# Attention in steps of four heads instead of two, with the PSUM banks, the rings of q and k and the place of the transposes rearranged, in an attention + MLP + experts kernel

## The reference

```python
# 1. attention with a causal window of 128 and a linear bias for each head
scores = q @ k.T / sqrt(64)
rel = pos[:, None] - pos[None, :]
scores = where((rel >= 0) & (rel < 128), scores - slope[h] * abs(rel), -1e9)
attn = exp(scores - max(scores)); attn /= sum(attn) + 1e-9
x = attn @ v                                   # 2304 x 512
# 2. MLP, d_ff = 2048
h = x @ w_in
x = (h * clip(h + 3, 0, 6) / 6) @ w_out
# 3. each token goes to one of 8 experts (cosine similarity with an embedding), d_ff = 1024
out[t] = gate[t] * (max(x[t] @ w1[e], 0) @ w2[e])
```

## Time and profile before

| | |
|---|---|
| three runs | 952.06, 955.26, 955.92 us |
| the profiled execution | 952.92 us, of which the span from first to last instruction is 951.2 us |
| PE busy | 898.1 us (94%) |
| DVE busy | 505.7 us (53%) |
| ACT busy | 439.2 us (46%) |
| POOL busy | 233.4 us (25%) |
| granted TensorE clock, mean | 0.991 of full |
| first `up` of the MLP | 35.67 us from the start of the span |
| last `values` of the attention | 552.44 us |

### The profile page before, as it was taken

How to read it: one execution, slowest core, us unless ns; L and a number is a source line. 1 busy time by engine, 2 the same in 40 slices (tenths; PEclk the granted TensorE clock), 3 DMA queues, 4 the chain that set the end, 5 groups by cost and what they waited for, 6 DMA issues and landing times.

```text
span 951.2 us, 17668 instructions
## 1 busy us (share of the span) xinstructions
PE 898.1 (94%) x5821; PEld 745.7 (78%) x5821; DVE 505.7 (53%) x1537; ACT 439.2 (46%) x1203; POOL 233.4 (25%) x247
## 2 busy tenths in 40 slices
PE   5799999899999999999999999799999999999996
PEld 3678888787788887787888889676788888888885
DVE  6755448566566665565665554678355345435100
ACT  4577545454445544545545433372344333344441
POOL 5464000000000000000000010036556556655532
PEclk9899999999999999999999999999999999999999
DMA  8542411101211101112100000366545544543100
GB/s 188 135 133 74 144 34 34 45 7 24 57 34 34 45 8 45 34 35 56 23 7 23 1 24 1 113 198 203 173 128 166 178 123 146 185 128 112 38 22 10
DMA packets 83415, 75.39 MB, mean 79 GB/s; under 512 B 61736, under 2 KB 61736, under 8 KB 83202
## 3 DMA queue, kind: packets, MB, share of 16 engines
q1 hardware_dynamic: 78754, 61.94, 22.9%
q0 software_dynamic: 4000, 11.29, 3.8%
q10 hardware_dynamic: 576, 1.05, 0.4%
HBM read 64.80 MB, written 11.30 MB: 80 GB/s over the span
## 4 chain that ended last, share of the span: by engine, by line
PE 87%; DVE 5%; ACT 2%; issue 2%; DMA 1%; POOL 1%; POOLq 0%; SPq 0%; ACTq 0%; DVEq 0%
PE ps_h L712 21%; PE ps_y L727 20%; PE ps_h L831 14%; PE ps_s L864 14%; PE ps_s L663 4%; PE ps_stage_out L696 4%; PE ps_t L675 4%; PE ps_y L855 2%; PE ps_stage_out L647 1%; PE ps_t L804 1%; ACT gated_hi L985 1%; DVE dot_junk L1170 1%; DVE arena L1130 1%; DMA arena<-in_k 1%; DVE row_den L1139 1%
## 5 line engine op out<-in xcount | busy, mean ns | idle before, releaser
L712 PE MATMUL ps_h<-x_hi,win_hi 128*128 128x256 f32 x576 | 175.3, 304 | 1.6 <-DVE x_lo L1159 1.6
L712 PE MATMUL ps_h<-x_lo,win_hi 128*128 128x256 f32 x576 | 164.0, 285 | 0.0
L712 PE MATMUL ps_h<-x_hi,win_lo 128*128 128x256 f32 x576 | 163.9, 285 | 0.0
L1191 DVE TENSOR_TENSOR gated_lo<-gated,gated_hi 128x256 fp32r<-128x256 f32 x144 | 62.9, 437 | 132.5 <-ACT gated_hi L985 132.1
L985 ACT CAST gated_hi<-gated 128x256 fp32r<-128x256 f32 x144 | 58.4, 406 | 153.9 <-PE ps_y L727 135.2
L981 ACT ACTIVATE clip<-ps_h,half 128x256 f32<-128x256 f32 x144 | 68.6, 476 | 121.4 <-PE ps_h L712 121.0
L727 PE MATMUL ps_y<-wout_hi,gated_hi 128*128 128x512 f32 x288 | 115.0, 399 | 2.1 <-issue 2.1
L712 PEld LDWEIGHTS ps_h<-x_hi,win_hi 128*128 128x128 f32 x576 | 111.0, 193 | 5.1 <-DVE x_lo L1159 2.0
L543 POOL MEMSET arena<- 128x128 bf16 x1 | 0.2, 204 | 464.9 <-DVE x_lo L1159 464.9
L727 PE MATMUL ps_y<-wout_hi,gated_lo 128*128 128x512 f32 x288 | 113.9, 396 | 0.0
L727 PE MATMUL ps_y<-wout_lo,gated_hi 128*128 128x512 f32 x288 | 112.5, 391 | 0.0
(11 more groups left out here) (197 smaller groups left out, 1729.4 us busy)
## 6 DMA issues: line engine op xcount, KB each, us to landing
arena<-in_moe_w SPq DMA_DIRECT2D x64, 512.0 KB
y_scratch<-y_sb SPq DMA_DIRECT2D x9, 512.0 KB, 3.7
arena<-in_v SPq DMA_DIRECT2D x16, 256.0 KB, 2.9
en_all<-in_moe_w_out SPq DMA_DIRECT2D x16, 256.0 KB, 2.8
arena<-in_q SPq DMA_DIRECT2D x15, 256.0 KB, 3.2
arena<-in_k SPq DMA_DIRECT2D x15, 256.0 KB, 3.9
en_all<-in_moe_w_in SPq DMA_DIRECT2D x12, 256.0 KB, 3.1
en_all<-en_scratch SPq DMA_DIRECT2D x1, 2048.0 KB, 10.0
```

What stands on the lines that cost most here:

```text
L712: last = pe.matmul(ps_h[m % 2][:, 0:TB], a[:, c, w], r[:, c, x], start=n == 0, stop=n == 3 * KC - 1)
L1191: dve.tensor_tensor(gl[m % 2][:], gate[:], gh[m % 2][:], ALU.subtract).then_inc(dve_gl, 1)
```

## The change

A step is now one group and four heads (`q4`, half of the eight): 40 steps instead of 80.

- **Banks.** The staged heads fill the bank `ps_stage` (four transposes), the outputs have the bank `ps_out` (256 columns). The transposes of `prob`, now two banks full, go into the banks of the scores, `ps_s` (in the first four steps into the MLP's `ps_h`). So `values` no longer waits for the stage copy, nor `stage` for `x_lo`; `scores(s)` waits for `take_pT(s-2)` and `transposes(s)` for DVE to have read the scores of step s + 1.
- **Depth.** `OUT` is 2 instead of 3 and `prob` has two buffers instead of three. `transposes(it-1)` stands in the same iteration as `normalise(it-1)`; before, it was one iteration behind it.
- **Order.** From iteration 5 (the new `FIRST`) to 40 there are 3.5 slots to an iteration: 16 of 3, 16 of 4, and one each of 1, 2, 5 and 6. PE does `values`, `scores`, two slots, `transposes`, `stage`, the other slots. DVE does one slot (with its router passes) ahead of `normalise`. ACT does two exponentials, a slot, two exponentials, a slot, and then `take_pT` and `stage_copy`. In iterations 0 to 4 PE does `values(it-2)`, `scores(it)`, `stage(it+1)`, `transposes(it-1)`.
- **Loads.** q and k come four heads at a time into rings of three. POOL splits two weight pieces for each normalised step instead of one. The embedding's small work moves to iterations 7 and 10.

```diff
-    STEPS = NG * NP
+    NQ = NP // 2
+    STEPS = NG * NQ
-    NEGS, OUT = 3, 3
+    OUT = 2
...
-    EMB_AT, EN_AT = FIRST + 4, FIRST + 8
-    EARLY = FIRST - OUT
-    ALONE = FIRST
+    EMB_AT, EN_AT = FIRST + 2, FIRST + 5
+    EARLY = FIRST - 1
+    ALONE = 2 * FIRST
...
-                    reach(pool, dve_n, 2 * n)
+                    reach(pool, dve_n, n // 2)
...
             def stage(s):
-                if s - OUT > EARLY:
-                    pe.wait_ge(dve_xl, s - OUT)
+                reach(pe, act_stage, s)
...
             def scores(s):
-                reach(pe, dve_s, 2 * s)
+                reach(pe, dve_s, 4 * s)
+                reach(pe, act_t, s - 1)
...
             def transposes(s):
-                pe.wait_ge(dve_n, 2 * s + 2)
+                pe.wait_ge(dve_n, s + 1)
                 reach(pe, act_t, s)
+                if s >= EARLY:
+                    pe.wait_ge(dve_s, 4 * min(s + 2, STEPS))
...
             def values(s):
                 pe.wait_ge(act_t, s + 1)
-                if s < EARLY:
-                    reach(pe, dve_xl, s - 1)
-                else:
-                    pe.wait_ge(act_stage, min(s + OUT, STEPS - 1) + 1)
-                    if s + OUT >= STEPS:
-                        pe.wait_ge(dve_xl, s)
+                reach(pe, dve_xl, s)
...
                 if it < STEPS:
                     scores(it)
-                if 0 <= it - OUT + 1 < STEPS:
-                    transposes(it - OUT + 1)
-                for m in mine[:1]:
+                for m in mine[:2]:
                     slot(m)
-                if it + 1 < STEPS:
+                if it + 1 < STEPS and it < FIRST:
                     stage(it + 1)
-                for m in mine[1:]:
+                if 0 <= it - 1 < STEPS:
+                    transposes(it - 1)
+                if it + 1 < STEPS and it >= FIRST:
+                    stage(it + 1)
+                for m in mine[2:]:
                     slot(m)
...
+                for m in mine[:1]:
+                    slot(m)
                 if 0 <= it - 1 < STEPS:
                     normalise(it - 1)
-                for m in mine:
+                for m in mine[1:]:
                     slot(m)
```

More of the change, by code:

```diff
@@ L233, in _program @@
         bias = part(H * 3 * P // 2, (H, 3 * P), BF16)
-        prob = [part(4 * P, (2, 2 * P)) for _ in range(NEGS)]
+        prob = [part(8 * P, (4, 2 * P)) for _ in range(2)]
         pT = [part(4 * P, (2, 2, P)) for _ in range(2)]
@@ L634, in stage @@
             def stage(s):
-                g, i, p = place(s)
+                g, i, q4 = place(s)
                 R = rows(g)
@@ L649, in stage @@
+                for j in range(2):
+                    if s == 0 and j == 0:
+                        pe.wait_ge(ld_pair, 32)
+                    elif j == 0 or s == 0:
+                        pe.wait_ge(ld_qk[s % 3], 32 * (s // 3 + 1))
+                    for n, src in enumerate((k_nat, q_nat)):
+                        last = pe.transpose(ps_so[:, (2 * n + j) * P:(2 * n + j) * P + R],
+                                            src[s % 3][0:R, 2 * j:2 * j + 2, :], ident[0:R, 0:R])
                 last.then_inc(pe_stage, 1)
@@ L666, in transposes @@
[L666 to L676 removed]
+                for j in range(2):
+                    for c in (0, 1):
+                        n = min(P, at + w - c * P)
+                        if c * P < at or n <= 0:
+                            continue
+                        for hh in range(2):
+                            d = slice(hh * D, (hh + 1) * D)
+                            last = pe.matmul(ps_s[hh][0:R, (2 * j + c) * P:(2 * j + c) * P + n],
+                                             qkT[d, 2 * NP + j, 0:R], qkT[d, 2 * (2 * q4 + j) + c, 0:n],
+                                             start=True, stop=True)
@@ new lines, in scores, with transposes @@
+                last.then_inc(pe_s, 1)
+            def transposes(s):
+                g, i, q4 = place(s)
+                R = rows(g)
+                pe.wait_ge(dve_n, s + 1)
+                reach(pe, act_t, s)
+                if s >= EARLY:
+                    pe.wait_ge(dve_s, 4 * min(s + 2, STEPS))
+                for j in range(2):
+                    for hh in range(2):
+                        for kg, w in chunks(g):
+                            c = kg % 2
+                            last = pe.transpose(turned_in(s)[j][0:w, (2 * hh + c) * P:(2 * hh + c) * P + R],
+                                                prob[s % 2][0:R, 2 * j + hh, c * P:c * P + w], ident[0:R, 0:R])
@@ L952, in take_pT @@
+                for j in range(2):
+                    bank = turned_in(s)[j]
+                    src = bank[:].rearrange("p (h j r) -> p h j r", h=2, r=P)
+                    if i and R == P:
+                        last = act.copy(pT[j].rearrange("p h j r -> p (h j r)"), bank[:])
+                    else:
+                        for kg, w in chunks(g):
+                            last = act.copy(pT[j][0:w, :, kg % 2, 0:R], src[0:w, :, kg % 2, 0:R])
                 last.then_inc(act_t, 1)
@@ L1147, in take_x @@
+                last.then_inc(dve_n, 1)
             def take_x(s):
-                g, i, p = place(s)
-                bank, at = out_of(s)
+                g, i, q4 = place(s)
+                src = ps_t[:, 0:2 * P].rearrange("p (j r) -> p j r", j=2)
                 if s < EARLY:
@@ L1152, in take_x @@
                     for cols, own in ring(g):
-                        last = dve.tensor_copy(xh[:, p, cols], bank[:, at + own.start:at + own.stop])
+                        last = dve.tensor_copy(xh[:, 2 * q4:2 * q4 + 2, cols], src[:, :, own])
                     last.then_inc(dve_xh, 1)
@@ L1365, in finish_gates @@
                 dve.reciprocal(gate_tok[:, t0:t1], total[:, t0:t1]).then_inc(dve_gate, 1)
-            scored = []
-            for s in range(STEPS):
-                scored.append((scored[-1] if s else 0) + 2 * len(chunks(place(s)[0])))
             for it in range(LASTK + 1):
```

212 lines of the change are left out of this document (96 added, 116 removed).

## The result

The changed kernel takes 970.5 us (median of four runs, 966.35 to 971.08), the kernel before 955.4 us (952.06 to 955.92) beside it: a ratio of 1.0156 (1.0119 to 1.0193), 15.1 us slower. The profiled execution of after took 966.35 us, with a span of 964.5 us where before had 951.2: 13.3 us more. The forecast was 962, 7 us slower, with a range to 973; the sign and the range hold, the size is half of what came. The traces are compared by their spans.

The account below looks back on a forecast made before the run. The prediction took PE, busy 94% of the span, as the bound. Losses of 48.3 us less gains of 40.2 made it 8 us slower, taken as 7 on the median 955.3: 962 us, range 948 to 973.

Parts of the forecast that it names:

- Gain 2: PE's attention matmuls in the loop: half the changes of kind go, saving 12.6 us (0 to 20).
- 2 (loss 2 does not come): Rival: transposes hardly wait for DVE in the loop, 15 of 20 us go; 947 us, chance 0.13.
- 4 (gain 2 only moves): Rival: the fixed parts between PE's kinds of matmul are moved, not saved; 12.6 us more, 975, chance 0.05.
- loss 2: In the loop, PE's transposes now wait for DVE's normalise, costing 20 us (5 to 25).
- loss 3: Smaller waits, 8.5 us: iteration 5's two `up`, POOL in iterations 5 to 8, ACT's tables, values in 14 and 32.
- loss 4: Low clock after the start-up and after the waits in iterations 5 and 14, costing 7 us (2 to 15).
- gain 3: Clock falls of the kernel before, one of 2.9 us and one of half that, go: 4.4 us saved.
- the sign that I named for being wrong: Whole run: the prediction is wrong if more than four low-clock stretches appear.
- Rival 3: In the loop, the clock falls after waits over 1 us with transposes behind; some 11 us, 973, chance 0.1.
- Loss 1: Start-up: one closed chain through DVE, PE and ACT brings the first `up` at 48.5 us; costs 12.8 (8 to 15).
- Rival 1: The clock holds at 2.4 GHz from the start-up on; first `up` at 43.8 us, 950 in all, chance 0.17.
- Gain 1: In the loop, PE's waits of values for ACT's stage copy, put down to a shared bank, go: 20.8 us saved.

Follow-up runs that it names:

- Experiment 2: Changed kernel with only the router passes of an iteration's first slot put behind normalise on DVE, its gate and low part staying ahead; 952.27 us.
- experiment 1: Changed kernel with DVE doing normalise ahead of all slots, as in the kernel before; 937.04 us.
- Experiment 7: Changed kernel with POOL's two subtractions for the first slot of iterations 5 to 8 waiting until normalise is done; 958.56 us.
- experiment 10: Changed kernel with unused f32 transposes of the identity filling PE's idle time in start-up iterations 1 to 4; 962.72 us.
- experiment 9: Changed kernel with 12 unused identity matmuls filling PE's idle time in each of start-up iterations 1 to 4; 961.85 us.
- experiment 8: Changed kernel with one wait put back on PE: values waits for the stage copy of two steps later, banks staying apart; 970.89 us.
- experiment 5: Kernel before, with stage and stage_copy ahead of the slot on PE and ACT in iterations with one slot; 953.09 us.
- Experiments 1 and 6: The second: as experiment 1, and in iterations 0 to 4 PE does scores ahead of values, DVE take_x after normalise; 929.25 us.

## Why the prediction was right and where it was not

**What held.** The frame did: the start-up 12.7 us longer (12.8 said), the stage copy's wait gone, and the new wait of `transposes` in 23 places, 0.27 to 0.4 in most and 5.0 once. From start to start the waits of the loop, without those of iterations 5 to 8, cost 19.8 us (20.0 said). The way there is the part to keep: the wait was built from rows of before for each kind of slot, and then counted over the slots as they are dealt. Experiment 2 confirms that it is the router passes (the loop is 16.2 us shorter without them in front), experiment 1 that it is DVE's order (33 us, with what follows). Gain 2 came in as well: 1.02, 1.10 and 1.33 us from start to start for sixteen values, sixteen scores, and transposes with the stage. Experiment 1 shows the gains on the whole: with the new wait out of the way, the loop is 32.2 us shorter than before. Of the rivals, 2 (loss 2 does not come) and 4 (gain 2 only moves) are ruled out by this.

**What failed: the size of loss 3.** "In iterations 5 to 8 POOL's subtractions hold up DVE: 2." That was 0.5 us for each iteration, half of what one row sum lost beside a subtraction. Measured: the four multiplications of each lost 1.8 us (3.06 instead of 1.25), 7.2 in all, and nothing of it was covered. DVE reaches `normalise` at the moment at which ACT's piece lets POOL go (68.56 and 68.74), and POOL then issues two subtractions in a row. Put into the sum, 7.2 for 2 makes it 13.3 us slower, and the spans show 13.3. That it fits to a tenth is luck: the third item of loss 3, `values` waiting for `take_pT` in iterations 14 and 32, had 2.5 us and shows 0.3 us of idle time in each, while loss 4 was too small by about as much. "From the first `up` to the last `values` some 6 us less than before" fails with the same step (it is 0.2 us more), and the 6 was not the sum's own, which has 4.7. Experiment 7 is the test: with POOL's pieces behind `normalise` the multiplications take 1.14 us, and the idle time ahead of the four transposes is 7 us less; their remaining 1.96 and 1.70 us are the 2 and 2 that the sum had for the two `up` in a row and for ACT's tables. The error was one of place. The row with the contention stood in the trace (1.15 us instead of 0.16), and the prediction took it for the small operation that it happened to hit, where the changed order put four large ones.

**Loss 4, the clock.** The sum had 7 us for the low stretches of after against 4.4 for those of before, and named four stretches as the limit. There are more. In the loop (the columns are those of the stretches above):

```profile
56.00:62.00 6.00, 5.54 (x30) 5.22 (x30) 1.58 (x5) 3.44 (x8) 2.51 (x2) 0.72 0.52 132
104.00:110.00 6.00, 5.48 (x29) 5.02 (x30) 1.60 (x5) 2.29 (x6) 0.58 (x3) 0.72 0.19 44
176.00:182.00 6.00, 5.55 (x30) 5.32 (x30) 2.88 (x9) 2.51 (x6) 0.00 (x0) 0.72 0.19 44
191.00:197.00 6.00, 4.21 (x26) 3.81 (x28) 1.35 (x6) 1.63 (x4) 0.00 (x0) 0.50 0.04 8
```

They follow the waits of 3.84, 3.58, 2.24 and 4.98 us. In this kernel none follows one of 1.58 us or less. With the first 3 us behind the first `up`, and each 3 us counted as (1 - clock) times PE's busy time, the loop of after loses some 9 us to the clock and that of before some 4.5, an estimate from such windows. (The 1.37 us of gain 3 is 1.33 by its own terms, which changes nothing.) So the term was near, but the sign that I named for being wrong did appear, and two of the four stretches are loss 3's again: longer waits that brought falls, gone in experiment 7. Rival 3, a fall after every wait of over 1 us with transposes behind it, is wrong as it stood: of its six waits one brought a fall here, that of 2.24 us at 176, and experiment 10 speaks against its reason. It is not empty either: in experiment 9's kernel one wait of 1.58 us, at 81 us, was followed by a fall, where the changed kernel's was not. In the kernel before, the second fall followed a wait of only 0.97 us, with one of 0.55 us behind it:

```profile
171.06 0.44 PE L647 MATMUL ps_stage_out<-ident,arena 128*128 128x128 f32 x2 [0.97 <-DVE x_lo L1159]
```

```profile
173.00:176.00 3.00, 3.00 (x20) 2.78 (x17) 2.00 (x10) 1.15 (x4) 0.00 (x0) 0.50 0.38 87
```

In the loops of these traces a wait of 2.23 us or more of idle time was always followed by a fall, and one of between 0.97 and 2.06 us at times; what decides is open.

**Loss 1, the start-up, was right by its middle, and in part by luck.** 48.5 was chosen between 43.8 at the full clock and 50.9 at the low one. Both ends can now be seen: with fillers the first `up` comes at 42.2, and in experiment 8, whose start-up is that of the changed kernel, at 50.7. There the last full turn took 10.2 us (10.6 said) from the transposes at 33.44; in experiment 9 it took 7.5 (8.0 said). So of the 12.7 us, 6.5 are the closed chain and 6.2 the clock, if the fillers changed nothing but the clock. The changed kernel's own start-up lies between the levels, and its place there differs from one execution to the next: the same start-up ended between 48.41 and 50.76 us in five traces, so 48.5 met the shortest of them, and the loss is 12.7 to 15.1 us. Rival 1 did not come: a start-up with fillers ran at 2.4 GHz, but the change's own bursts of values and scores did not keep it there.

**Gain 1 was right in size and wrong in its reason.** The prediction put the wait down to the shared bank. Experiment 8 shows that the new order alone removes it; experiment 5 shows that the old kernel could not have it that way, since its stage would wait for `x_lo` instead.

**What was not seen.** That the loss was a choice of the order on DVE and not of the four heads. The prediction priced that order at 20 us and never asked what the kernel would take without it. Experiments 1 and 6 are the answer: 16 and 24 us faster than before.

## What to carry to other kernels

When a dependent step is moved one iteration closer, write down the producer's queue ahead of it, instruction by instruction, and price the consumer's wait against it; then move the producer to the front of its queue, since work that has slack, here the slots' passes, can stand behind it. If two engines were once seen to slow each other, look up which of their instructions meet in the new order, and multiply by those, not by the one that met before. A chain that passes through several queues opens only when every queue on it is reordered.

## What the runs showed of the hardware

**DVE and POOL on SBUF take turns.** One f32 multiplication of 128x256 took 0.35 us alone (experiment 7) and up to 1.35 us beside POOL's f32 subtractions of 128x512 (1.27 us each); four took 3.06 instead of 1.14 to 1.25, and still 2.92 with subtractions of half the size. The Trainium skill, "SBUF — State Buffer", in "SBUF: two separate sides", describes the port pair that VectorE and GpSimd share as an exclusive lock, held for a whole instruction by whichever starts first; for VectorE it names instructions in a 2-port mode or with two inputs in SBUF, and these multiplications have one beside the scalar of each row. The durations agree with the lock (which mode VectorE was in, no trace shows), and they add that cutting the other's instruction did not help where more were queued behind it.

**A granted clock of 1.00 can be a missing record.** Experiment 8's kernel, PE in its start-up, and the granted clock (third number from the end) in the same stretch:

```profile
46.77 1.97 PE L701 MATMUL ps_out<-arena 128*64 128x128 f32 x16 [1.16 <-ACT arena L964]
48.67 2.08 PE L667 MATMUL ps_s<-arena 64*128 64x128 f32 x16
```

```profile
44.00:50.00 6.00, 4.84 (x36) 4.11 (x36) 0.85 (x2) 1.36 (x4) 3.34 (x4) 1.00 0.33 95
```

Sixteen scores in 2.01 us are what they take at 1.2 GHz, and the column reads 1.00 in every stretch of that kernel from 17 to 53 us. The kept trace of this run holds no clock record before 53.0 us, and the view counts time without a record as full. In the changed kernel, whose records begin at 23.6 us, and whose transposes at 25 us ran at the full level (four in 0.66 us), it reads 0.67 for 26 to 29 us and 0.50 for 35 to 38. In experiment 10 they begin at 22.0 us, ahead of the stretch read there. In a start-up the level is read from the durations of known matmuls, and the mean clocks of two runs are compared only where their records begin alike.

**Idle time can cost twice.** Ahead of the first `up` 6.2 of the 12.7 us lost went with the low level, and 12 matmuls more in each of four turns took them away.
